# Rotating staging quarters, and weight, statistic and root work in other places of a fused attention and two-MLP kernel

## What is computed

```python
attn = softmax(where(mask, q @ k.T / 8, -1e9)) @ v     # local mask for heads 0-3, strided for heads 4-7
x = attn.transpose(0, 2, 1, 3).reshape(B, S, 512)
h = gelu(x @ w_in); u, v = h[..., :512], h[..., 512:]
v_n = (v - mean(v)) / sqrt(var(v) + 1e-6) * g_ln
x = x + (u * (einsum('ts,bsd->btd', w_sg, v_n) + b_sg)) @ w_out
xn = (x - mean(x)) / sqrt(var(x) + 1e-6) * g_ln2
out = x + maximum(xn @ w_ch1, 0) @ w_ch2                # w_ch1 512 x 2048, w_ch2 2048 x 512
```

## Time and profile before

| | us |
|---|---|
| median of three runs | 711.6 |
| the profiled execution's own time | 710.58 |
| its span | 708.8 |
| PE (TensorE matmul) busy | 668.1 (94%) |
| PEld (its weight loads) busy | 628.4 (89%) |
| DVE (VectorE) busy | 549.3 (78%) |
| ACT (ScalarE) busy | 355.7 (50%) |
| POOL (GpSimd) busy | 249.9 (35%) |

### The profile page before, as it was taken

One profiled execution on the slowest core, in us unless ns is written; L12 is line 12 of the kernel. 1 busy time (PEld: TensorE's weight loads), 2 busy tenths in 40 slices (PEclk: granted clock), 3 DMA queues, 4 the chain that ended last, 5 costly groups with the idle time before them and its releaser, 6 DMA issues.

```text
span 708.8 us, 14199 instructions
## 1 busy us (share of the span) xinstructions
PE 668.1 (94%) x5158; PEld 628.4 (89%) x5160; DVE 549.3 (78%) x1305; ACT 355.7 (50%) x894; POOL 249.9 (35%) x261
## 2 busy tenths in 40 slices
PE   7899999989998996999999989989898999999997
PEld 4569888989798975999999979889897999999997
DVE  6867976788688937998686785576789789797993
ACT  7655774577347823444563443243675444344441
POOL 1368232425161426568326336322101412312121
PEclk9999999999999997999999999999999999999999
DMA  8560007000610042118253657758881552625401
GB/s 296 224 221 8 2 2 291 5 2 2 252 60 1 2 142 78 54 52 299 81 177 111 201 203 233 250 191 286 256 253 55 202 182 96 256 84 204 166 18 50
DMA packets 49012, 98.26 MB, mean 139 GB/s; under 512 B 4656, under 2 KB 32176, under 8 KB 46256
## 3 DMA queue, kind: packets, MB, share of 16 engines
q1 hardware_dynamic: 48240, 96.16, 39.0%
q0 software_dynamic: 704, 1.21, 0.7%
HBM read 64.83 MB, written 32.52 MB: 137 GB/s over the span
## 4 chain that ended last, share of the span: by engine, by line
PE 61%; issue 15%; DMA 9%; DVE 8%; POOL 3%; ACT 3%; SPq 1%; DVEq 0%; POOLq 0%; ACTq 0%
PE pair L1619 9%; PE pair L1621 9%; PE pair L1620 9%; PE pair L1828 9%; PE pair L1830 8%; PE pair L1829 8%; DMA hid_scratch<-stage 4%; DVE stage L1482 3%; PE pair L1676 3%; PE pair L1643 3%; PE pair L1658 2%; DMA sums_scratch<-w_raw 1%; POOL xr L970 1%; DVE res L1348 1%; DMA f_raw<-w_ff_dram 1%
## 5 line engine op out<-in xcount | busy, mean ns | idle before, releaser
L1828 PE MATMUL pair<-xf_hi,w_hi 128*128 128x288 f32 x896 | 268.4, 300 | 14.1 <-ACT stage L1168 8.4
L1829 PE MATMUL pair<-xf_lo,w_hi 128*128 128x288 f32 x896 | 265.8, 297 | 0.0
L1830 PE MATMUL pair<-xf_hi,w_lo 128*128 128x288 f32 x896 | 265.0, 296 | 0.0
L1828 PEld LDWEIGHTS pair<-xf_hi,w_hi 128*128 128x128 f32 x896 | 169.3, 189 | 18.3 <-ACT stage L1168 10.1
L1830 PEld LDWEIGHTS pair<-xf_hi,w_lo 128*128 128x128 f32 x896 | 170.0, 190 | 0.0
L1829 PEld LDWEIGHTS pair<-xf_lo,w_hi 128*128 128x128 f32 x896 | 169.6, 189 | 0.0
L1482 DVE TENSOR_TENSOR stage<-pair,stage 128x576 f32<-128x576 f32 x136 | 100.7, 753 | 53.2 <-ACT stage L1168 30.4
L1084 ACT ACTIVATE xf_hi<-res 128x576 fp32r<-128x576 f32 x140 | 92.9, 681 | 95.2 <-PE pair L1830 54.0
L549 DVE TENSOR_TENSOR xf_lo<-res,xf_hi 128x576 fp32r<-128x576 f32 x140 | 109.2, 797 | 4.4 <-ACT xf_hi L1084 4.3
L970 POOL TENSOR_TENSOR xr<-xr,stage 128x576 f32<-128x576 f32 x16 | 36.3, 2266 | 166.6 <-DVE stage L1482 166.4
L1172 ACT ACTIVATE stage<-stage 128x576 f32<-128x576 f32 x64 | 43.4, 681 | 72.1 <-DVE stage L1482 72.1
(11 more groups left out here) (133 smaller groups left out, 1298.5 us busy)
## 6 DMA issues: line engine op xcount, KB each, us to landing
hid_scratch<-stage SPq DMA_DIRECT2D x64, 288.0 KB, 3.0
res<-hid_scratch SPq DMA_DIRECT2D x16, 1152.0 KB, 6.5
w_raw<-w_ff_dram SPq DMA_DIRECT2D x16, 512.0 KB, 3.9
v_sb<-vW_dram SPq DMA_DIRECT2D x16, 384.0 KB, 7.0
x_scratch<-res SPq DMA_DIRECT2D x4, 1152.0 KB, 5.6
xr<-x_scratch SPq DMA_DIRECT2D x16, 288.0 KB, 2.9
out_dram<-xr SPq DMA_DIRECT2D x16, 288.0 KB, 2.3
k_sb<-kT_dram SPq DMA_DIRECT2D x15, 304.0 KB, 6.7
```

The source lines that it names most:

```text
L1828: pe.matmul(dst, wh, xh, start=(start and x == 0), stop=False)
L1829: pe.matmul(dst, wh, xl, start=False, stop=False)
L1830: last = pe.matmul(dst, wl, xh, start=False, stop=(stop and x == n - 1))
```

## The change

Five edits, none of which adds or removes work of an engine.

1. The quarters of `stage` rotate from lockstep to lockstep (`STAGE_AT`): each of the four roles takes the quarter of the role that was freed one place earlier, so P1's copy takes the quarter that was stored first, the role of `c11` the second, of `u3` the third, of `c22` the fourth. The waits follow (`wait_stage`), in the output part on GpSimd's additions.
2. In the last period both `first_high` stand behind both `sum_hi`, both `split_first` behind both `centre`, `form_t3` between the two sums. In all periods the second statistic stands after `v_part` (2, 2) instead of (2, 1); in the period of batch 2 the second `normalise_x` stands between the two `centre`.
3. In the periods of batches 1 and 2 the fourth statistic stands after the first group of step t = 1, and its `copy_variance` ahead of the second `copy_pT` of that step.
4. In the hidden part `normalise_x` of half 0 moves to the end of lockstep q = 1, half 1 to q = 2 behind `u3`; GpSimd loads the variance, takes the roots and spreads them earlier.
5. In locksteps 12 to 15 both `first_high` stand behind `rectify(P4)`, the first `rest_high` ahead of `rectify(P3)`; VectorE's `split_rest` stands ahead of its two `split_first`.

```diff
@@ -99,6 +99,11 @@
 Y_ADDED = {P2: 1, P7: 2, P5: 3, P3: 4}
+Y_QUARTER = (1, 4, 2, 3)
+FREED_BY = (3, 0, 1, 2)
+STAGE_AT = [tuple(range(4))]
+for _m in range(B * LOCKSTEPS + B - 1):
+    STAGE_AT.append(tuple(STAGE_AT[-1][i] for i in FREED_BY))
@@ -358,6 +363,17 @@
+        def stage_at(m, i):
+
+            return stage[:, :, STAGE_AT[m][i], :]
+
+        def wait_stage(engine, m, i):
+
+            if m > B * LOCKSTEPS:
+                engine.wait_ge(y_added, 4 * (m - 1 - B * LOCKSTEPS) + Y_QUARTER[FREED_BY[i]])
+            elif m >= 1:
+                engine.wait_ge(hid_stored[FREED_BY[i]], 16 * m)
+
         def output_at(i):
@@ -674,7 +690,7 @@
                 sp.wait_ge(hid_ready, 4 * m + done)
-                sp.dma_start(hid_dram[n, i, :, 2 * q:2 * q + 2, :], stage[:, :, i, :]).then_inc(hid_stored[i], 16)
+                sp.dma_start(hid_dram[n, i, :, 2 * q:2 * q + 2, :], stage_at(m, i)).then_inc(hid_stored[i], 16)
@@ -943,8 +959,6 @@
                         form_t3(pool, B + 2 * q - 1)
-                    if norm and q == 1:
-                        invert_roots(n + 1)
                     for i in range(P2, FORMS):
@@ -958,16 +972,18 @@
                             store_variance(n + 1)
-                        if norm and q == 0 and i == P5:
+                        if norm and q == 0 and i == P7:
                             load_variance(n + 1)
-                        if norm and q == 1 and i == P7:
+                        if norm and q == 0 and i == P4:
+                            invert_roots(n + 1)
+                        if norm and q == 1 and i == P6:
                             spread_rstd(n + 1)
...
                 pool.wait_ge(xr_in[i], 16 * (n + 1))
-                pool.tensor_tensor(output_at(i), output_at(i), stage[:, :, i, :], ALU.add).then_inc(y_added, 1)
+                pool.tensor_tensor(output_at(i), output_at(i), stage_at(m, i), ALU.add).then_inc(y_added, 1)
@@ -1093,8 +1109,9 @@
                         sum_hi(4 * n + h)
-                        if last:
-                            first_high(h)
+                if last:
+                    for g in range(2):
+                        first_high(g)
                 if norm and not last:
@@ -1124,6 +1141,8 @@
                         sum_hi(4 * b - 1)
+                    if b >= 1 and t == 1:
+                        copy_variance(b - 1, 1)
                     if 1 <= t <= QUADS:
@@ -1132,8 +1151,8 @@
                         round_gated(b, 2 * t)
-                    if b >= 1 and t < 2:
-                        copy_variance(b - 1, t)
+                    if b >= 1 and t == 0:
+                        copy_variance(b - 1, 0)
@@ -1161,15 +1180,12 @@
                 wait_product(act, m, P1)
-                if m <= B * LOCKSTEPS:
-                    wait_past(act, hid_stored[1], 16 * m)
-                else:
-                    act.wait_ge(y_added, 4 * (m - B * LOCKSTEPS))
-                act.activation(stage[:, :, 1, :], product_at(m, P1), ACT.Copy).then_inc(p1_copied, 1)
+                wait_stage(act, m, 1)
+                act.activation(stage_at(m, 1), product_at(m, P1), ACT.Copy).then_inc(p1_copied, 1)
...
                 act.wait_ge(drained, m * FORMS + DRAINED[product])
-                act.activation(stage[:, :, i, :], stage[:, :, i, :], ACT.Relu).then_inc(hid_ready, 1)
+                act.activation(stage_at(m, i), stage_at(m, i), ACT.Relu).then_inc(hid_ready, 1)
@@ -1201,9 +1217,8 @@
                     form_high(following + 4)
-                if last:
-                    first_high(UNITS + 2 * q)
-                    first_high(UNITS + 2 * q + 1)
+                if last and q >= 1:
+                    rest_high(UNITS + 2 * q - 2)
                 rectify(m, P3, 1)
@@ -1213,12 +1228,15 @@
                     form_high(following + 5)
-                if last and q >= 1:
-                    rest_high(UNITS + 2 * q - 2)
                 rectify(m, P4, 2)
+                if last and q == 3:
+                    form_high(following + 6)
+                if last:
+                    first_high(UNITS + 2 * q)
+                    first_high(UNITS + 2 * q + 1)
                 if last and q >= 1:
                     rest_high(UNITS + 2 * q - 1)
-                if q == 3:
+                if q == 3 and not last:
                     form_high(following + 6)
@@ -1377,11 +1395,13 @@
                         sum_chunks(dve, 4 * n + h)
-                        if n == 1:
-                            normalise_x(0, h)
+                        if n == 1 and h == 0:
+                            normalise_x(0, 0)
                         split_sum(dve, 4 * n + h)
-                    for h in range(2):
-                        centre(n, h)
+                    centre(n, 0)
+                    if n == 1:
+                        normalise_x(0, 1)
+                    centre(n, 1)
                 norm_all_v(b, first)
@@ -1411,11 +1431,13 @@
                     sum_chunks(dve, r + h)
+                    if h == 0:
+                        form_t3(dve, 0)
                     split_sum(dve, r + h)
-                    split_first(dve, h)
-                form_t3(dve, 0)
                 for h in range(2):
                     centre(b - 1, h)
+                for g in range(2):
+                    split_first(dve, g)
                 norm_all_v(b)
@@ -1478,30 +1500,24 @@
                 else:
-                    to, x = stage[:, :, dst, :], stage[:, :, src, :]
+                    to, x = stage_at(m, dst), stage_at(m, src)
                 dve.tensor_tensor(to, product_at(m, i), x, ALU.add).then_inc(drained, 1)
-
-            def wait_stage(m, i, product):
-                if m <= B * LOCKSTEPS:
-                    wait_past(dve, hid_stored[i], 16 * m)
-                else:
-                    dve.wait_ge(y_added, 4 * (m - 1 - B * LOCKSTEPS) + Y_ADDED[product])
...
                 dve.wait_ge(p1_copied, m + 1)
-                wait_stage(m, 0, P2)
+                wait_stage(dve, m, 0)
                 combine(m, P2, 0, 1)
...
             def u3(m):
-                wait_stage(m, 2, P7)
+                wait_stage(dve, m, 2)
                 combine(m, P7, 2, 1)
...
                 combine(m, P5, 1, 1)
-                wait_stage(m, 3, P5)
+                wait_stage(dve, m, 3)
                 combine(m, P5, 3, 2)
@@ -1532,8 +1548,6 @@
                     centre(B - 1, m - 5)
-                if n == 2 and q == 2:
-                    normalise_x(n + 1, 0)
                 if q == 3:
@@ -1541,12 +1555,10 @@
                     split_first(dve, EARLY + 2 * q + 1)
-                if n == 1 and q == 2:
-                    normalise_x(n + 1, 0)
                 if q == 3:
...
                 u3(m)
-                if n == 2 and q == 2:
+                if norm and q == 2:
                     normalise_x(n + 1, 1)
@@ -1562,13 +1574,13 @@
                     split_rest(dve, EARLY + 2 * q)
-                if n == 1 and q == 2:
-                    normalise_x(n + 1, 1)
+                if norm and q == 1:
+                    normalise_x(n + 1, 0)
+                if last and q in (1, 2):
+                    split_rest(dve, UNITS + 2 * q - 2)
                 if last:
...
                     split_first(dve, UNITS + 2 * q + 1)
-                if last and q in (1, 2):
-                    split_rest(dve, UNITS + 2 * q - 2)
                 if last and q == 3:
@@ -1759,7 +1771,7 @@
                     v_part(b, s, (k,), first)
-                    if b >= 1 and (k, s) in ((1, 2), (2, 1)):
+                    if b >= 1 and (k, s) in ((1, 2), (2, 2)):
                         statistic(4 * (b - 1) + k - 1)
@@ -1782,8 +1794,8 @@
                         group(b, NGELU + 2 * t + j, first)
-                    if b >= 1 and t == 1:
-                        statistic(4 * b - 1)
+                        if b >= 1 and t == 1 and j == 0:
+                            statistic(4 * b - 1)
...
                 projections(b, last=True)
```

## The result

The changed kernel takes 687.9 us in the median of four executions (687.53 to 690.06), the kernel before 710.94 us in the median of four (710.09 to 711.71); the ratio is 0.968 with a 95% interval from 0.966 to 0.971. It is faster, and the forecast was 688.7 us. The profiled execution of after is the slowest of its four, 690.06 us with a span of 688.2 us; the profiled one of before took 710.58 us with 708.8.

A forecast was written before the change was run, and what follows sets the result against it. TensorE, busy 94% of the span, was taken to bound the kernel. Gains of 3.2 + 1.0 + 6.6 + 12.3 + 1.5 = 24.6 us, less 1.7, took the median from 711.6 to 688.7 us; range 679 to 700 us.

The forecast's parts named there:

- Edits 1 and 4, locksteps 0 to 11: Second MLP, locksteps 0 to 11: copies and additions no longer wait for stores; gain 12.3 us (8 to 13.3).
- Edit 2, the last period: Last period: the statistic's wait goes, the mix starts 6.9 us earlier behind a new 3.2 us wait; gain 6.6 us.
- 0.3 us for VectorE's lag: Start of the mix: allowance for VectorE reaching its first gate 2 us after TensorE's first mix group; 0.3 us lost.
- 1.7 for the half clock: Start of the mix: one stretch of half clock behind the new 3.2 us wait; 1.7 us lost.
- The lock of the shared port pair: Last period: if VectorE and GpSimd exclude each other, each new meeting costs in full; gain only 3 us, not 6.6.
- Edits 2 and 3, batches 1 and 2: Periods of batches 1 and 2: three waits for statistics go; gain 4.2 us, from 3.2 and 1.0.
- the 1.6 us for each batch: Periods of batches 1 and 2: gain from the earlier fourth statistic, 1.6 us each, bounds 0 and 2.06.
- Edits 1 and 5, the end: Locksteps 12 to 15 and output: most of a 4.1 us loss goes, the output takes some back; gain 1.5 us.
- cover gone: Rival, whole kernel: VectorE and the transfers bind where the waits were; 699.3 us, chance 0.22.
- The rotation does nothing: Rival, locksteps 0 to 11: additions are late for other reasons, these locksteps give 3 us; 698.0 us, chance 0.11.
- All goes: Rival, whole kernel: all the named losses vanish, with 9 us in the last period; 680.1 us, chance 0.11.
- The slower one: Rival, locksteps 12 to 15: late weights make first_high ahead of copy_p1 hold up TensorE; slower, chance 0.04.

The follow-up runs named there:

- v_chain_first: The changed kernel with, in the last period, GpSimd's split_all_v ahead of two weight sums and the first weights' splitting behind the v chain; 685.12 us, ratio 0.9635.
- firsts_early_15: The changed kernel with both first_high of lockstep 15 ahead of rectify(P3) and VectorE's split_form(fill + 4) ahead of its split_first there; 685.45 us, ratio 0.9634.
- weights_not_moved: The changed kernel with edit 5 undone, the last weights' splitting in its earlier order; 693.28 us, ratio 0.9742.
- store_ahead_of_load: The changed kernel with the store of quarter 3 ahead of a weight load on SyncE in locksteps 8 and 10; 690.38 us, ratio 0.9706.
- reload_later: The changed kernel with the reload of hidden quarter 2 of batch 0 issued in lockstep 10 instead of 9; 689.12 us, ratio 0.9657.

## Why the prediction was right, and where it was not

**The total** was right by 0.8 us (688.7 against 687.9), and the traces say that some of this is luck: in the profiled executions the gain was 20.5 where 22.9 was forecast.

**Edits 1 and 4, locksteps 0 to 11:** right in mechanism and size, 12.2 us against 12.3. The stores no longer hold up the copy (27.2 us in 11 places to 1.7 in one), and 137.1 us lie in the 136 to 138 named beforehand. How the gain divides depends on what goes in first. With the rotation first it is 11.3 us and then 0.9 for all the rest (rotation alone 138.0, all 137.1). With edits 2 to 5 first it is 4.3 us (145.0 without the rotation; edits 2 and 3 alone have 147.2), and then 7.9 for the rotation.

**Edit 2, the last period:** the chain was right to 0.1 us. The first `v_norm` was forecast 17.0 us after the period's start (274.1 less 321.80 - 64.69 = 257.1) and came at 271.83 - 254.79 = 17.0. The mix was to start 6.9 us earlier and started 7.0 earlier, with a wait of 2.99 us for `vn_lo`, where 3.2 was forecast. `v_chain_first` shows that its cause is the one named, GpSimd's roots behind its weight sums: with the roots 4.6 us earlier the wait is gone. What was mis-sized is what followed, 0.3 us for VectorE's lag and 1.7 for the half clock, 2.0 in all; the mix took 17.56 instead of 14.84 us, 2.7.

**The lock of the shared port pair** (the Trainium skill, SBUF — State Buffer, section "SBUF: two separate sides") was to bring the gain down to 3 us. The rows agree with the rule for pairs: the last `vn_lo` took 2.44 us beside `split_rest`, the four before it 1.28 to 1.30, and in `v_chain_first`, beside the shorter `split_first`, the last took 1.66. But the chain from the first `v_norm` to the last `vn_lo` took 284.77 - 271.83 = 12.9 us against 13.3 before, with the same single long `vn_lo` at its end (2.47 us before): this meeting was in it before the change as well, and the three more that the lower bound supposed did not come about. The rule prices a meeting; it doesn't say that there are more of them.

**Edits 2 and 3, batches 1 and 2:** 4.2 us forecast, 3.1 measured, inside the bounds of 0 to 5.1. The two waits of 2.06 us and the one of 1.04 us are gone. The term that was too large is the 1.6 us for each batch: batch 1 gained 1.15 us (73.50 to 72.35), batch 2 1.97 (74.80 to 72.83), and 1.0 of that was set down for the second statistic. The moved copy now holds up a matmul itself, 0.61 us in batch 2 (0.13 before), and further on the engines hold TensorE up for 0.79 and 0.72 us where it hadn't waited. TensorE's timeline:

```profile
215.95 0.28 PE L1670 MATMUL pair<-eye_f,probs 96*128 96x96 f32 x1 [0.61 <-ACT rstd_a L1072]
...
249.24 0.40 PE L1633 MATMUL pair<-gated_hi,wout_lo 128*128 128x288 f32 x1 [0.72 <-issue]
```

**Edits 1 and 5, the end:** 1.5 us forecast, 1.7 measured, as a sum of 2.6 gained and 0.9 lost. The order was right, and so was the wait of about 3 us at the output, behind ScalarE's two rectifications and two forms: VectorE idled 3.10 us there and TensorE 2.67, and `firsts_early_15` takes it away. What I didn't see is that edit 5 is needed by the rotation. I weighed it against the 4.1 us of the kernel before, and undone it costs 4.2 to 5.4 us. One reading was off besides: the prediction has the late copy of lockstep 14 come through the rectification's store. In the kernel before that store landed at 501.30, ScalarE worked without a gap from `first_high` at 496.96 to the copy at 501.68, and so its own queue ended last. The sum isn't touched, since it went by that queue.

**The start** was 0.8 us later in the profiled execution, where no edit lies. It started at 107.7 to 110.9 us in the other kernels of this study, so it is scatter of single executions.

Of the rivals, "cover gone" had 3 us for the last period and 10 for the locksteps, where 4.3 and 12.2 were measured. "The rotation does nothing" fell with 137.1 us and with the 9.6 us that it gains alone. "All goes" fell with the wait at the mix. The slower one did not happen: no matmul of the changed kernel waits for ScalarE's copy (two weight loads do, 0.4 us in all). Its mechanism exists, though, in `weights_not_moved`.

## What to carry to other kernels

When a store's latency decides whether a buffer is free, change which buffer is filled next rather than how fast it is stored: let the quarter stored first be the first that is wanted. Then look for what else stood in the old wait's shadow: here the order of the last weights cost 4 to 5 us under the rotation. In these runs an instruction that waited for a transfer held up what was queued behind it, on SyncE and GpSimd as much as on VectorE: `store_ahead_of_load` freed a store and held up a load that a weight sum, and through it VectorE, was waiting for. Work that has slack, such as GpSimd's weight sums, goes behind a chain that an engine is waiting for, even if it is ready first.

## What the runs showed that I had not expected

**The same wait costs different amounts.** Nine kernels of this study start the mix behind a wait of 2.9 to 3.0 us for the same `vn_lo`. In their profiles the mix took 14.91 us (three of them), 16.46 or 16.47 (four) and 17.56 or 17.66 (two), against 14.84 without the wait. The clock shows it; the window from 280 to 290 has 0.70 in after (above), 0.83 in `firsts_early_15` and 1.00 in `reload_later`, at nearly the same busy time and place:

```profile
280.00:290.00 10.00, 7.02 (x42) 6.81 (x41) 9.93 (x13) 2.36 (x5) 3.96 (x3) 0.83 0.28 93
```

```profile
280.00:290.00 10.00, 7.00 (x54) 7.01 (x54) 9.93 (x14) 2.00 (x4) 3.25 (x2) 1.00 0.30 93
```

In all nine the instructions of every engine up to the mix are the same and in the same order, since edits 1, 4 and 5 and the later tries lie behind it. So a stretch of half clock behind a wait of this size isn't a fixed price but one of 0.1 to 2.8 us, and two executions of one kernel can differ by as much. What decides between them no run here tells. It is one reason not to believe a difference of 1 to 3 us between two profiled executions without the medians beside it.

**One profiled execution can lie 4 us from the others.** In `reload_later` the profiled one took 684.97 us and the rest 688.96 to 689.74, in the changed kernel 690.06 against 687.53 to 687.99. The stages' lengths above are exact for their own execution, and only that.
